# Query and key blocks turned by VectorE instead of TensorE, attention products one place later, and a later w_in split, in a fused attention and two-layer feed-forward kernel

## What is computed

```
scores = q @ k^T / 8 - slope[h] * dist          # kept: 8 global keys, and 96 local keys behind the query
a      = softmax(scores over the kept keys);   attn = a @ v
x      = attn as (tokens, heads * 64)          # 3072 x 512
h      = x @ w_in ;   g = h * cos(h);   y = g @ w_out          # layer 1
h2     = relu(y @ w2_in) ; out = (h2 * h2) @ w2_out            # layer 2
```

## Time and profile before

| | us |
|---|---|
| median of 3 runs | 1262.38 |
| profiled execution | 1262.92 |
| its span on the chip | 1261.1 |
| TensorE busy | 1231.7 (98%) |
| GpSimd busy | 617.8 (49%) |
| VectorE busy | 704.4 (56%) |
| ScalarE busy | 564.0 (45%) |

### The profile page before, as it was taken

The page is one execution under the profiler, slowest core; times in us unless marked ns, Lnnn a source line. Parts: engine busy times, 40 slices in busy tenths (PEclk is TensorE's granted clock), DMA queues, the critical chain, the costliest instruction groups (busy, mean ns, idle before and its releaser), DMA issues.

```text
span 1261.1 us, 18119 instructions
## 1 busy us (share of the span) xinstructions
PE 1231.7 (98%) x6240; PEld 993.3 (79%) x6240; DVE 704.4 (56%) x1434; ACT 564.0 (45%) x1164; POOL 617.8 (49%) x687
## 2 busy tenths in 40 slices
PE   5789999999999999999999999999999999999998
PEld 3667777777777777777888888888888888888887
DVE  6478777777777767777778942323223323222222
ACT  4656667666666666666533322222222222222221
POOL 4767565665655666655534433333333333333332
PEclk9889999999999999999999999999999999999999
DMA  4533234333433333342136541131131131321211
GB/s 122 158 104 87 78 112 131 91 90 102 132 107 92 122 91 103 98 144 81 34 111 206 141 139 51 51 116 43 51 117 50 47 112 50 105 64 46 80 50 59
DMA packets 150949, 118.80 MB, mean 94 GB/s; under 512 B 63680, under 2 KB 115008, under 8 KB 150848
## 3 DMA queue, kind: packets, MB, share of 16 engines
q1 hardware_dynamic: 150848, 117.55, 31.6%
HBM read 96.54 MB, written 20.97 MB: 93 GB/s over the span
## 4 chain that ended last, share of the span: by engine, by line
PE 94%; DVE 2%; POOL 2%; ACT 1%; issue 1%; DMA 0%; DVEq 0%; SPq 0%; POOLq 0%; ACTq 0%
PE psum L555 15%; PE psum L556 14%; PE psum L557 14%; PE psum L574 7%; PE psum L581 7%; PE psum L576 7%; PE psum L580 7%; PE psum L579 7%; PE psum L575 7%; PE psum L646 3%; PE psum L610 3%; PE psum L631 2%; PE psum L591 1%; POOL probs L486 1%; ACT probs L766 1%
## 5 line engine op out<-in xcount | busy, mean ns | idle before, releaser
L471 POOL TENSOR_SCALAR w_out_hi<-w_out_raw 128x512 fp32r<-128x512 f32 x192 | 138.9, 724 | 581.5 <-PE psum L581 312.5
L555 PE MATMUL psum<-x_parts,w_in_hi 128*128 128x512 f32 x768 | 308.3, 401 | 0.0
L556 PE MATMUL psum<-x_parts,w_in_hi 128*128 128x512 f32 x768 | 300.4, 391 | 0.0
L557 PE MATMUL psum<-x_parts,w_in_lo 128*128 128x512 f32 x768 | 300.2, 391 | 0.0
L473 POOL TENSOR_TENSOR w_out_lo<-w_out_raw,w_out_hi 128x512 fp32r<-128x512 f32 x192 | 261.9, 1364 | 16.0
L1012 DVE TENSOR_TENSOR g_lo<-act_a,g_hi 128x512 fp32r<-128x512 f32 x192 | 139.7, 728 | 184.9 <-ACT g_hi L807 181.6
L797 ACT ACTIVATE hs<-psum 128x512 f32<-128x512 f32 x96 | 57.4, 598 | 359.9 <-PE psum L557 359.9
L555 PEld LDWEIGHTS psum<-x_parts,w_in_hi 128*128 128x128 f32 x768 | 144.7, 188 | 34.6 <-issue 6.7
L557 PEld LDWEIGHTS psum<-x_parts,w_in_lo 128*128 128x128 f32 x768 | 144.6, 188 | 31.3
L556 PEld LDWEIGHTS psum<-x_parts,w_in_hi 128*128 128x128 f32 x768 | 145.0, 189 | 27.7
L574 PE MATMUL psum<-g_hi,w_out_hi 128*128 128x512 f32 x384 | 157.6, 411 | 1.5 <-issue 1.5
(11 more groups left out here) (76 smaller groups left out, 1641.3 us busy)
## 6 DMA issues: line engine op xcount, KB each, us to landing
w_out_raw<-in_moe_w_out_dram SPq DMA_DIRECT2D x192, 256.0 KB, 2.7
vals<-in_v_dram SPq DMA_DIRECT2D x80, 112.0 KB
w_stage<-in_moe_w_in_dram SPq DMA_DIRECT2D x32, 256.0 KB, 2.9
w_dram<-w_stage SPq DMA_DIRECT2D x16, 512.0 KB, 3.1
raw<-in_k_dram SPq DMA_DIRECT2D x96, 64.0 KB, 2.5
raw<-in_q_dram SPq DMA_DIRECT2D x96, 64.0 KB, 2.2
y_dram<-y_stage SPq DMA_DIRECT2D x24, 256.0 KB, 3.5
x_raw<-y_dram SPq DMA_DIRECT2D x6, 1024.0 KB, 5.1
```

What stands on the lines that cost most here:

```text
L555: pe.matmul(to, hi, x[:, 0, c], start=(c == 0), stop=False)
L556: pe.matmul(to, hi, x[:, 1, c], start=False, stop=False)
L557: last = pe.matmul(to, lo, x[:, 0, c], start=False, stop=(c == KC - 1))
```

## The change

- `load_qk` issues eight DMAs of 32x8x32 elements a group instead of four of 128x2x64. Each fills 32 partitions of `raw` with eight 32x32 blocks side by side, 256 elements in one run for each partition.
- `transpose_qk`, `copy_qk` and bank 6's part in them are gone. `turn_qk(G)` on VectorE transposes all 32x32 blocks, one instruction of 128x256 for k and one for q, and writes straight into `kq`. It stands at the head of VectorE's list in each pair, and ahead of `reduces` in the lead-in.
- `move_globals` (GpSimd) makes the small copy of the global keys, for r = 0.
- `attend(G-2)` stands behind `scores(G)`, where `attend(G-1)` stood at the end of the pair. `low_x` moves behind `reduces`, `round_x` behind `front`.
- Banks: scores and turned probabilities use 6 and 7, attention's output 5, the hidden chunk only 4 (5 is no longer used in turn), so `up(F)` waits for `front(F-1)`.
- Five chunks of w_in are split in the lead-in (EARLY), eleven around pairs 0 to 5; `split_w2` begins with pair 6.

```
-        raw = sb("raw", [P, 3, 2, 2, 2 * D])
+        raw = sb("raw", [P, 3, 2, PAD])
...
-            return 7 if G < AHEAD - 1 else 6
+            return 7 if G < AHEAD - 1 else 5
 
         def hidden_bank(F):
-            return 2 + F if F < 2 else 4 + F % 2
+            return 2 + F if F < 2 else 4
...
-        W2_FROM = 4
+        W2_FROM = 6
+        EARLY = 5
...
                 for i, src in enumerate((k, q)):
                     for h in range(2):
-                        rows = src[b, 2 * j + h, PAD * r:PAD * r + PAD]
-                        sp.dma_start(raw[:, G % 3, i, :, D * h:D * h + D], rows.rearrange("(t p) d -> p t d", p=P))\
-                          .then_inc(qk_loaded[G % 3], 16)
+                        rows = src[b, 2 * j + h, PAD * r:PAD * r + PAD].rearrange("(n p) (a d) -> a p n d", p=32, a=2)
+                        for a in range(2):
+                            at = 64 * h + 32 * a
+                            sp.dma_start(raw[at:at + 32, G % 3, i].rearrange("p (n d) -> p n d", d=32), rows[a]).then_inc(qk_loaded[G % 3], 16)
...
+            def move_globals(G):
+                b, r, j = place(G)
+                if r == 0:
+                    pool.wait_ge(qk_turned, G + 1)
+                    pool.tensor_copy(kq[:, j].rearrange("p (a n) -> p a n", a=2)[:, :, 0:GLOB],
+                                     kq[:, j, None, K_AT:K_AT + GLOB].to_broadcast((P, 2, GLOB))).then_inc(globals_moved, 1)
...
                 for p in range(L1_PAIRS):
-                    if p < 3:
-                        split_in(AHEAD + 2 * p)
+                    if EARLY + 2 * p < FC:
+                        split_in(EARLY + 2 * p)
                     pair(p, True)
-                    if p < 2:
-                        split_in(AHEAD + 2 * p + 1)
+                    if EARLY + 2 * p + 1 < FC:
+                        split_in(EARLY + 2 * p + 1)
...
-                if F >= 4:
-                    pe.wait_ge(h_copied, F - 1)
+                if F >= 3:
+                    pe.wait_ge(h_copied, F)
...
                 if window and G < GROUPS:
                     scores(G)
+                if window and 0 < p and G - 2 < GROUPS:
+                    attend(G - 2)
                 down(F, window)
-                if window and G + 1 < GROUPS:
-                    transpose_qk(G + 1)
...
+            def turn_qk(G):
+                b, r, j = place(G)
+                dve.wait_ge(qk_loaded[G % 3], 128 * (G // 3 + 1))
+                if r > 0:
+                    dve.wait_ge(tails_moved, tails(G))
+                elif G >= PAIRS:
+                    dve.wait_ge(scores_ready, 2 * (G - PAIRS + 1))
+                dve.transpose(kq[:, j, K_AT:G_B], raw[:, G % 3, 0])
+                dve.transpose(kq[:, j, Q_AT:Q_AT + PAD], raw[:, G % 3, 1]).then_inc(qk_turned, 1)
...
-                if window and p > 0 and G - 2 < GROUPS:
-                    low_x(G - 2)
+                if window and G + 1 < GROUPS:
+                    turn_qk(G + 1)
                 if F + 2 < STEPS:
                     angle(F + 2)
                 if window and G < GROUPS:
                     reduces(G)
+                if window and p > 0 and G - 2 < GROUPS:
+                    low_x(G - 2)
```

More of the change, by code:

```diff
@@ L227, in v_count, with starts @@
             return 16 * sum(v_dmas(n) for n in range(G % 3, G + 1, 3))
+        def starts(G):
+            return sum(place(n)[1] == 0 for n in range(G + 1))
         def tails(G):
@@ L494, in pair @@
                     move_tail(G + 1)
+                    move_globals(G + 1)
                 if F + 3 < STEPS_ALL:
@@ L582, in down @@
                     last.then_inc(down_done, 1)
-            def transpose_qk(G):
-                pe.wait_ge(qk_loaded[G % 3], 64 * (G // 3 + 1))
-                if 0 < G <= AHEAD:
-                    pe.wait_ge(qkT_copied, G)
-                if G > AHEAD:
-                    pe.wait_ge(scores_biased, 4 * (G - 1) + 2)
-                for n in range(4):
-                    last = pe.transpose(psum[:, T_BANK, P * n:P * n + P], raw[:, G % 3, n // 2, n % 2], ident[:])
-                last.then_inc(qk_transposed, 1)
             def scores(G):
                 b, r, j = place(G)
-                pe.wait_ge(qkT_copied, G + 1)
+                pe.wait_ge(qk_turned, G + 1)
+                if r == 0:
+                    pe.wait_ge(globals_moved, starts(G))
                 if 2 <= G < AHEAD:
                     pe.wait_ge(scores_biased, 4 * (G - 1))
-                if G >= AHEAD:
+                if G == AHEAD:
                     pe.wait_ge(x_lo_ready, G - 1)
+                if G > AHEAD:
+                    for s in probsT_copied:
+                        pe.wait_ge(s, G - 1)
                 for ti in range(2):
@@ L665, in pair @@
                 down(F + 1, window)
-                if window and G - 1 < GROUPS:
-                    attend(G - 1)
             pe.wait_ge(consts_set, 3)
             def window():
-                transpose_qk(0)
                 for G in range(AHEAD - 1):
                     scores(G)
-                    transpose_qk(G + 1)
                     if G >= 2:
@@ L681, in window @@
                 scores(AHEAD - 1)
-                transpose_qk(AHEAD)
                 turn_probs(AHEAD - 3)
@@ L700, in each @@
                             i, t = divmod(4 * r + n, T)
-                            last = pe.transpose(psum[:, T_BANK, P * n:P * n + P], gen_raw[:, i, t], ident[:])
+                            last = pe.transpose(psum[:, GEN_T_BANK, P * n:P * n + P], gen_raw[:, i, t], ident[:])
                         last.then_inc(gen_transposed, 1)
@@ L820, in pair @@
                     copy_out(i - 1)
+                if F + 3 < STEPS_ALL:
+                    front(F + 3)
                 if window and p > 0 and G - 2 < GROUPS:
                     round_x(G - 2)
-                if F + 3 < STEPS_ALL:
-                    front(F + 3)
                 if window and G < GROUPS:
                     exps(G)
-                if window and G + 1 < GROUPS:
-                    copy_qk(G + 1)
                 if 2 <= s < 6 and i < 2 * TILES - 1 and (i >= TILES - 1 or not window):
@@ L849, in window @@
                 act.wait_ge(consts_set, 2)
-                copy_qk(0)
                 for G in range(AHEAD - 1):
-                    copy_qk(G + 1)
                     exps(G)
@@ L858, in window @@
                 round_x(AHEAD - 4)
-                copy_qk(AHEAD)
                 exps(AHEAD - 1)
@@ L1048, in window @@
             def window():
+                turn_qk(0)
                 biases(0)
                 for G in range(AHEAD - 1):
+                    turn_qk(G + 1)
                     reduces(G)
@@ L1060, in window @@
                 low_x(AHEAD - 4)
+                turn_qk(AHEAD)
                 reduces(AHEAD - 1)
```

49 lines of the change are left out of this document (18 added, 31 removed).

## The result

The changed kernel takes 1274.19 us (median of four, 1272.79 to 1274.28) against 1262.70 in the same comparison: a ratio of 1.0087, interval 1.0069 to 1.0104. It is slower by 0.9%, clear of the noise; the forecast was 1253.3 (range 1244 to 1267). The profiled execution's span went from 1261.1 to 1272.3 us.

What follows compares the result with a forecast made beforehand. It took TensorE's own list as the bound from 98 to 615 us, and whoever feeds it before. Terms 0 - 15.4 - 3.3 + 3.3 + 4.3 + 1.5 = -9.6 on 1262.92 gave 1253.3 us, range 1244 to 1267.

Steps and rivals of the forecast that it cites:

- the ring: GpSimd (tail, normalise, split) to VectorE (turn, reduces, invert): would pace lead-in groups 4 to 9, 3 us at most.
- Transposes, -15.4: TensorE's list, pairs 1 to 35: dropping the four transposes and their changeover saves 0.44 us a pair, 15.4 in all.
- Attend, -3.3: TensorE: attend beside scores saves one changeover to or from large matmuls, 0.09 in 37 pairs, 3.3 us (0 to 6.7).
- Lead-in: SyncE's list before the pairs: q and k issues at 0.43 each, last landing at 58.8, up(0) near 65.8, +1.9 us.
- dear issues: Rival, lead-in: each of the eight q and k issues costs 0.51 like before, +6.4 us, 1259.7 in all; chance 0.20.
- The slack in a pair: Pairs with r > 0: turn waits for GpSimd's tail until 2.8, second front ends at 12.9, 1.4 us to spare.
- Behind a split of layer 2's weights, +3.3: In 11 odd pairs with r > 0 between 7 and 35, late normalise stalls 0.3 us each: +3.3 (0 to 9).
- Pairs 4 and 5, +4.3: Behind two splits of w_in, stalls of 0.7 us in pair 4 and 3.6 in pair 5: +4.3 (2 to 7).
- Tile ends, +1.5: up(16i) needs x whose low_x now stands behind the reduces: 0.5 us in pairs 6, 22 and 30, +1.5 (0 to 4).
- late VectorE: Rival: turn waiting for GpSimd's tail makes the second front late in 24 pairs, single bank passes it on; 1276; chance 0.18.
- lighter: Rival: q and k issues at 0.35 us and both attend changeovers saved, -3 - 3.4, 1247 in all; chance 0.14.
- late landings: Rival, lead-in: DMAs on 32 partitions land much later than 2.2 us, 1262 to 1268 in all; chance 0.06.

Runs made afterwards that it cites:

- tail_early: The changed kernel with GpSimd's copy move_tail issued one pair earlier, ahead of split_out; 1249.45 us, ratio 0.9896 to the kernel before.
- tail_attend_old: tail_early with attend back at the end of the pair, two hidden banks and low_x at the head of VectorE's list; 1257.57 us, ratio 0.9956 to before.
- attend_old: The changed kernel with attend back at the pair's end, two hidden banks and low_x at the head of VectorE's list; 1278.72 us, ratio 1.0125 to before.
- before_8: The kernel before with q and k loaded by eight DMAs a group instead of four, TensorE still transposing; 1272.88 us, ratio 1.0085.
- tail_act: tail_early with q's four DMAs a group issued from ScalarE's queue instead of SyncE's in the lead-in; 1244.76 us, ratio 0.9853 to the kernel before.

## Why the prediction was wrong, point by point

The profiled execution took 1274.1 us, 20.8 more than forecast, and `up(0)` came at 75.09: past the 70 that the prediction named as a sign of being wrong.

From before to after `up(5)` moved by 7.6 us, and `attend(10)`, 1.0, now stands behind it instead of ahead: lead-in and pair 0 cost 8.6, predicted 0. From there to `up(80)` it is +2.4, predicted -9.6. tail_early splits that: without the ring -21.1 (predicted -18.7 for transposes and attend), and the ring +23.5 (predicted +9.1 in three places). So the miss is 8.6 in the lead-in and pair 0 and 14.4 in the ring, less 2.4 that the rest came out better. That -21.1 lies so near -18.7 is luck: attend gave more than twice its term, and the late splits took some of it back in pairs 1 to 5, for which the prediction has no term outside the ring.

- **Transposes, -15.4.** The price is right: 0.47 a pair instead of 0.44. Between `up(5)` and `up(80)` tail_attend_old gains 13.1 us over before and not 35 x 0.47 = 16.5, since its pairs 1 and 3 to 5 take 0.2 to 0.5 more than before.
- **Attend, -3.3.** Right sign, too small: -8.9. I took one changeover where the row gave two; the upper bound, 6.7, was the better value, and still 2.2 short.
- **Lead-in.** The price of an issue was 0.49 as a rule and 0.51 in the mean of the 80 (some were held up), not 0.43. This is the rival "dear issues": the last load that the lead-in waits for had landed at 65.27 instead of 58.8, 6.5 late; the rival had 6.4. I had weighed the form in SBUF by an analogy with the w_in row, against the row of the same tensor. The other 2.8 us come behind the landing: 9.8 to `up(0)` instead of 7.0, of which some 2.6 are three steps of TensorE at the lower clock. The bound of "3 us at most" for the ring of GpSimd and VectorE was wrong in kind: it hid behind SyncE and cost 12.2 - 3.0 = 9.2 us once SyncE's list had been shortened.
- **Pair 0.** Right: `up(5)` came 30.95 us after `up(0)`, predicted 30.4, or 31.6 with the 1.2 added for the lower clock.
- **The slack in a pair.** This is the failed step, beside the price of an issue in the lead-in. I let GpSimd's split of w_out begin at 0.1, right behind the last `down`, as if nothing held GpSimd up, and so put the turn at 2.8. But `normalise` ends when VectorE lets it begin; it now began at 414.07, 13.5 into the pair, against 9.6 in pair 22 before (412.93, the pair's start at 403.31), and the split began 1.7 into the next. I computed one trip around the circle from the old start times, and did not put the result in again. Turn at 4.0 and 5.9, 0.2 us lost even in the plain pairs (14.22 against 14.04).
- **Behind a split of layer 2's weights, +3.3.** Pair 9 lost 1.4 (15.48 against 14.04) where I had 0.3. Over the 11 odd pairs the changed kernel takes 11.1 us more than tail_early, past the upper bound of 9. This is the largest part of the ring's miss.
- **Pairs 4 and 5, +4.3.** Measured 3.7 and 3.9 over 14.28, and 0.9 in pair 6: 8.5. The cheap r = 0 group of pair 4 did not help, `normalise` was already late.
- **Tile ends, +1.5.** Pairs 22 and 30 took 15.16 and 15.30 where tail_early has 14.04 and 13.83: 1.1 and 1.5 each, not 0.5. In tail_early no such wait is left, so they belong to the ring, not to `low_x`'s place by itself. Against tail_early the ring's 23.5 us are 8.7 in pairs 4 to 6, 11.1 in the odd pairs, 2.6 in pairs 22 and 30, and the small rest in the plain ones.
- **Layer 2, 0.** Right.
- **The rival "late VectorE"** had the mechanism and nearly the total, 1276. The total is luck: the rival had 31.9 us for the ring and nothing for the lead-in, measured are 23.5 and 8.6. It named the single bank as what hands the stall on, and 9.7 us of waits there bear that out; but attend_old shows that with two banks the stall only comes out elsewhere. I gave it 0.18 because its start, 4.2 us into the pair, lay 1.4 behind my estimate; the turn came at 4.0 and 5.9.
- **The rivals "lighter" and "late landings".** Both fall: the median issue of q or k cost 0.49 and not 0.35, and the last q of group 10 landed 1.8 us after its issue began, sooner than the 2.2 of before.
- **The two rules.** VectorE's transpose of 128x256 took 0.45 and 0.40 (0.77 from the start of the first to the end of the second, for 0.8 taken), like a subtraction of that size (0.42). Vector Engine (DVE) Microarchitecture Reference in the Trainium skill (3.8) has one element per cycle per lane, and these rows agree. The smaller packets were no bound here: the DMA share in the first 64 us was 0.48, below the 0.54 of before, and before_8, with as many issues and 256-byte pieces, has `up(0)` at 74.5 where the changed kernel has 75.1.

What stays open: why an issue of q or k costs 0.49 and one of v 0.31; the 0.03 to 0.09 a pair of attend, and why pairs 3 to 5 stay slow with the ring cut.

## What to carry to other kernels

When an in-order engine gets a new wait at the head of its list, write down who the releaser waits for. If the path leads back to the waiting engine, the slack of the old trace does not hold: go around the circle until the times stand still, or move the small releasing copy to where its inputs are ready. And a bound found by one trace hides the next: after cutting it, look for what now ends at the same time.

## What the runs showed of the hardware that was not expected

An issue of a DMA into `raw` cost 0.48 to 0.51 us on SyncE at 64 KB and at 32 KB, over 128 partitions or 32; cutting each transfer in two doubled the queue's time for q and k. ScalarE's queue took the same (tail_act, two issues):

```profile
51.12 0.97 ACTq L279 DMA_DIRECT2D raw<-in_q_dram  x2
```

In pair 4 of the changed kernel VectorE's `turns<-hs` began at 157.28, just after GpSimd's subtraction (157.21 to 158.49), and ended at 158.77: 1.49 us, where the same operation takes 0.42 at 162.00. It looks held until GpSimd was done. SBUF — State Buffer in the Trainium skill ("Who interferes with whom") says that the two share a pair of ports as a lock, and that the one issued second is blocked for the whole instruction; the row agrees. One such meeting took 1.07 us of VectorE (1.49 less 0.42).
